# Fused attention and two MLPs: the last tiles of probabilities, phi and v on 128 rows instead of 64

## The reference, cut to what matters

```python
q, k, v: (4, 8, 576, 64)
a = softmax(causal(q @ k.T / 8))                 # per head, 576 x 576
local = a @ v
q_p = where(q > 0, q, exp(q) - 1) + 1            # phi
mem_out = (q_p @ M_prev) / (q_p @ z_prev + 1e-6)
g = sigmoid(beta)                                # per head
attn = g * mem_out + (1 - g) * local
x = attn, heads side by side                     # (2304, 512)
x = (sigmoid(x @ w_gate) * (x @ w_val)) @ w_out  # 512 -> 1536 -> 512
h = x @ w_in                                     # 512 -> 2048
out = (h * clip(h + 3, 0, 6) / 6) @ w_out2       # (2304, 512)
```

## Time and profile before

| | |
|---|---|
| median of 3 runs | 1090.42 us (1088.56 to 1090.96) |
| time of the profiled execution | 1092.04 us |
| its span | 1090.2 us |
| TensorE matmuls, busy | 1066.3 us, 98% |
| TensorE weight loads, busy | 989.9 us, 91% |
| VectorE, ScalarE, GpSimd, busy | 698.4, 629.9, 543.9 us |
| chain that ended last, TensorE's share | 87% |

### The profile page before, as it was taken

The page is one execution under the profiler, slowest core; times in us unless marked ns, Lnnn a source line. Parts: engine busy times, 40 slices in busy tenths (PEclk is TensorE's granted clock), DMA queues, the critical chain, the costliest instruction groups (busy, mean ns, idle before and its releaser), DMA issues.

```text
span 1090.2 us, 20617 instructions
## 1 busy us (share of the span) xinstructions
PE 1066.3 (98%) x6784; PEld 989.9 (91%) x6784; DVE 698.4 (64%) x1521; ACT 629.9 (58%) x1414; POOL 543.9 (50%) x559
## 2 busy tenths in 40 slices
PE   5999999999999999999999999999999999999998
PEld 4668999999999999999999999988888888989887
DVE  5997757768756758767645444466578556664553
ACT  5787676776776767766754443465556343453333
POOL 5887567658766657765644654247881011000000
PEclk9999999999999999999999999999999999999999
DMA  8452442443443343343223335344544544454421
GB/s 187 126 141 65 116 107 65 118 112 82 110 111 94 94 123 95 95 124 96 60 68 97 88 107 175 117 150 140 187 170 148 173 116 119 117 175 121 117 59 58
DMA packets 123596, 125.98 MB, mean 116 GB/s; under 512 B 10352, under 2 KB 89712, under 8 KB 123248
## 3 DMA queue, kind: packets, MB, share of 16 engines
q1 hardware_dynamic: 123216, 121.15, 40.0%
q10 hardware_dynamic: 288, 3.67, 0.9%
HBM read 105.39 MB, written 19.40 MB: 114 GB/s over the span
## 4 chain that ended last, share of the span: by engine, by line
PE 87%; DVE 4%; DMA 2%; issue 2%; ACT 2%; POOL 2%; SPq 1%; DVEq 0%; POOLq 0%; ACTq 0%
PE ps L799 82%; PE ps L840 4%; PE ps L854 1%; DMA stage<-w_val 1%; DMA stage<-w_gate 1%; DVE prob L1536 1%; POOL prob L684 0%; DMA qk_st<-qk_t 0%; DVE q_s L1452 0%; ACT pt_hi L1136 0%; SPq L435 0%; DVE pt_lo L1484 0%; DVE Cb L1728 0%; DVE m_hl L1524 0%; POOL v_hl L651 0%
## 5 line engine op out<-in xcount | busy, mean ns | idle before, releaser
L799 PE MATMUL ps<-x_hi,WG 128*128 128x288 f32 x1536 | 324.2, 297 | 2.2 <-DVE pt_lo L1484 1.1
L799 PEld LDWEIGHTS ps<-x_hi,WG 128*128 128x128 f32 x1536 | 251.3, 188 | 5.2 <-issue 1.9
L799 PE MATMUL ps<-x_lo,WG 128*128 128x288 f32 x768 | 226.2, 295 | 0.0
L799 PE MATMUL ps<-XC,WC 128*128 128x384 f32 x1008 | 202.5, 336 | 2.1 <-DVE Cb L1728 1.7
L799 PEld LDWEIGHTS ps<-XC,WC 128*128 128x128 f32 x1008 | 180.3, 188 | 17.6 <-issue 3.2
L656 POOL TENSOR_TENSOR WG<-stage,WG 128x512 fp32r<-128x512 f32 x96 | 128.2, 1350 | 104.2 <-ACT WG L1164 104.2
L799 PE MATMUL ps<-wo,G_hi 128*128 128x512 f32 x540 | 168.1, 392 | 0.0
L799 PE MATMUL ps<-h_hi,WO 128*128 128x288 f32 x768 | 164.6, 297 | 0.2 <-DVE Y L1703 0.2
L684 POOL TENSOR_SCALAR prob<-prob,rscale 128x128 f32<-128x128 f32 (+4 forms) x160 | 110.9, 711 | 79.4 <-DVE rscale L1496 79.4
L799 PEld LDWEIGHTS ps<-x_lo,WG 128*128 128x128 f32 x768 | 144.3, 188 | 0.5
L1728 DVE TENSOR_TENSOR Cb<-ps,Cb 128x384 f32<-128x384 f32 x168 | 89.0, 554 | 83.3 <-PE ps L799 81.4
(11 more groups left out here) (137 smaller groups left out, 1971.2 us busy)
## 6 DMA issues: line engine op xcount, KB each, us to landing
WC<-w_in_parts SPq DMA_DIRECT2D x112, 256.0 KB, 2.7
stage<-w_out SPq DMA_DIRECT2D x64, 256.0 KB, 2.8
qk_st<-qk_t SPq DMA_DIRECT2D x54, 288.0 KB, 4.4
stage<-w_gate SPq DMA_DIRECT2D x48, 256.0 KB, 3.4
stage<-w_val SPq DMA_DIRECT2D x48, 256.0 KB, 3.3
w_in_parts<-WC SPq DMA_DIRECT2D x42, 256.0 KB, 2.0
qn_st<-q_n SPq DMA_DIRECT2D x16, 256.0 KB, 3.3
w_in_parts<-WC ACTq DMA_DIRECT2D x2, 1792.0 KB, 7.2
```

The costliest lines, as they stand in the source:

```text
L799: return pe.matmul(o, l, r, start=start, stop=stop, skip_group_check=True)
```

## The change

- In `turn_head` the last tile is turned as 128 rows. Each of the five outputs is 128 columns wide, but they still start 64 columns apart, so the second half of one is written over by the first half of the next. The copies out of PSUM read the same columns as before.
- In `turn_phi` the tail is turned as 128 rows. Its tile is now loaded with the last 128 tokens (64 of them for the second time), and what is used is the last 64 columns of the output.
- In `times_v_first` the last tile is multiplied on 128 rows. The rows 64 to 127 of that tile of both `v_first` buffers are cleared once at the start, on GpSimd, and SyncE waits for this (`v_zero`) ahead of the first load of v.
- The clearing of the last tile of `qn_st` is gone.

```diff
-        cleared = [v_st[:, QT - 1, :], qn_st[:, QT - 1, :]]
+        cleared = [v_st[:, QT - 1, :]]
...
             def load_phi(n):
-                load_tiles(qn_st, q_n, n, ld_phi)
+                head = q_n[bass.ds(n, 1), 0:(QT - 1) * P, :].rearrange("a (t p) c -> p (a t) c", p=P)
+                tail = q_n[bass.ds(n, 1), S - P:S, :].rearrange("a p c -> (a p) c")
+                sp.dma_start(qn_st[:, 0:QT - 1, :], head).then_inc(ld_phi, DMA)
+                sp.dma_start(qn_st[:, QT - 1, :], tail).then_inc(ld_phi, DMA)
...
                     for j in two:
                         load_m_first(0, j)
+                    sp.wait_ge(v_zero, 2)
                     load_tiles(v_first[0], v_n, 0, ld_v_first[0])
...
             for ap in cleared:
                 pool.memset(ap.bitcast(F32), 0.0).then_inc(init, 1)
+            for j in two:
+                pool.memset(v_first[j][:, QT - 1, :], 0.0).then_inc(v_zero, 1)
...
                 for k in range(i + 1):
-                    last = pe.transpose(ps[:, turn_bank(r, i), k * rows:(k + 1) * rows],
-                                        prob[odd][0:rows, p_off[i] + k * P:p_off[i] + (k + 1) * P], ident[0:rows, 0:rows])
+                    last = pe.transpose(ps[:, turn_bank(r, i), k * rows:k * rows + P],
+                                        prob[odd][:, p_off[i] + k * P:p_off[i] + (k + 1) * P], ident[:, :])
...
                 for t in (range(QT - 1) if j == 0 else [QT - 1]):
-                    rows = qrows[t]
                     o = t * P if j == 0 else P
-                    last = pe.transpose(ps[:, TURN if j == 0 else turn_bank(r, 0), o:o + rows], phi[0:rows, t, :], ident[0:rows, 0:rows])
+                    last = pe.transpose(ps[:, TURN if j == 0 else turn_bank(r, 0), o:o + P], phi[:, t, :], ident[:, :])
...
                 for k in tiles:
-                    rows = slice(0, qrows[k])
                     for a, b in ((0, P), (P, S)) if k == 0 else ((k * P, S),):
-                        last = mm(head_out(a, b), v_first[n % 2][rows, k, :], pt[rows, k, a:b], False, k == QT - 1)
+                        last = mm(head_out(a, b), v_first[n % 2][:, k, :], pt[:, k, a:b], False, k == QT - 1)
...
-                        (phit_hi[:, (QT - 1) * P:S], ps[:, turn_bank(r, 0), P:P + TAIL])
+                        (phit_hi[:, (QT - 1) * P:S], ps[:, turn_bank(r, 0), 2 * P - TAIL:2 * P])
```

More of the change, by code:

```diff
@@ L232, in attention_and_mlps @@
         ld_qk, ld_v, ld_phi, ld_m, ld_beta = [sem(x) for x in ("ld_qk", "ld_v", "ld_phi", "ld_m", "ld_beta")]
-        init, m_zero = sem("init"), sem("m_zero")
+        init, m_zero, v_zero = sem("init"), sem("m_zero"), sem("v_zero")
         g_e, g_1, g_r, gates = sem("g_e"), sem("g_1"), sem("g_r"), sem("gates")
@@ L1142, in move_phi @@
                 cols = slice(0, (QT - 1) * P) if i == 0 else slice((QT - 1) * P, S)
-                src = ps[:, TURN, 0:(QT - 1) * P] if i == 0 else ps[:, turn_bank(None, 0), P:P + TAIL]
+                src = ps[:, TURN, 0:(QT - 1) * P] if i == 0 else ps[:, turn_bank(None, 0), 2 * P - TAIL:2 * P]
                 act.activation(phit_first[:, cols], src, ACT.Copy).then_inc(moved_act, 1)
@@ L1473, in move_lo @@
                     cols = slice(0, (QT - 1) * P) if i == 0 else slice((QT - 1) * P, S)
-                    src = ps[:, TURN, 0:(QT - 1) * P] if i == 0 else ps[:, turn_bank(r, 0), P:P + TAIL]
+                    src = ps[:, TURN, 0:(QT - 1) * P] if i == 0 else ps[:, turn_bank(r, 0), 2 * P - TAIL:2 * P]
                     dst, hi = phit_lo[:, cols], phit_hi[:, cols]
```

## The result

The changed kernel takes 1085.23 us (median of 6 runs, 1083.96 to 1085.61), the kernel before 1090.29 us in the same comparison. The ratio is 0.9954, with a 95% interval of 0.9941 to 0.9967: 5.0 us faster, between 3.6 and 6.4. The forecast was 7.2 us and 1083.2 us; the gain is 0.7 of that. The time lies inside the wide range of 1079.5 to 1087, and 0.2 us outside of 1081.5 to 1085.0, the range of the forecast's own case.

The account below looks back on a forecast made before the run. TensorE was taken to bound the kernel, with VectorE also busy in the opening. 4.5 us from 97 us on plus 2.7 in the opening, 7.2 in all, off 1090.42 gave 1083.2 us; range 1079.5 to 1087.

Parts of the forecast that it names:

- the forecast's own case: Gaps go, saving 4.5 us from 97 us on and 2.7 in the opening; 1081.5 to 1085.0 us, 53 in 100.
- the two slower rivals: Small groups' gap stays, turns only lengthen: 1097.4 us, 4 in 100; turns wait for overlapping writes: 1103 us, 3 in 100.
- the opening gives nothing: First 97 us: VectorE's order of work sets the pace, TensorE only waits longer; 1085.9 us, 12 in 100.
- from 97 us on: After the opening: 23 heads at 0.09 and 11 phi tails at 0.24, less two waiting steps; 4.5 us.
- a later wait takes it back: Middle stage: ScalarE's waits for weights give each pair its 0.42 us back as waiting; about 1089 us, 8 in 100.
- The opening's term: First 97 us: 3.93 us of TensorE work from heads, phi and v, counted at TensorE's 68.6% chain share; 2.7 us.

Follow-up runs that it names:

- Experiments 1, 7 and 8: 1: only heads' turns on 128 rows, 1090.0 us; 7: VectorE's h_val ahead of a low part, kernel after, 1081.35 us; 8: same, kernel before, 1086.25 us.
- before_again: The kernel before run once more with no edit, for a second trace and as a measure of noise; ratio 0.9998 against itself.
- v alone: Only v's tail in the opening goes to 128 rows, with its clears and SyncE's wait, against the kernel before; 1089.5 us, ratio 0.9997.

## Why the prediction was right, and where it was wrong

The mechanism of the gain was right: small turns are shorter but each visit to 64 rows costs a gap of 0.29 to 0.30 us, and the change takes away one for each head, one for each pair (phi) and one for each tail of v in the opening. The prices were near: 0.07 us a head where 0.09 was forecast, 0.15 in the opening and 0.28 a pair in the middle stage for phi (0.24), 0.29 for v (0.24). Neither of the two slower rivals came true: the gap went, and overlapping writes cost at most the 0.004 us a turn between 0.115 and 0.111. Nor did "the opening gives nothing", though its 1085.9 is nearer to the 1085.23 than the forecast is: its repeating pairs got 0.57 us shorter. That the forecast is off by 2.0 us has other reasons.

Both terms of the sum came out smaller. The term "from 97 us on", 4.5 us, is 4.2 by the repeating distance, 2.2 to 4.6 by pairs of traces, and some 3.2 if the opening's 1.8 us are taken from the 5.0 of the runs. It rested on TensorE being busy for 477.53 of 480 us and on two places with a wait. Two things were wrong in this:
- A wait of 0.12 us on h_val stood in the repeating pairs and in no table of matmuls' waits: their records overlap, so a short idle time hides inside a busy share of 99%. It took the gain of one head of two, 0.08 us a pair, 0.9 us over eleven. Experiments 1, 7 and 8 show it. In a pair of the change it is half made up, for phi's part gained 0.30 us and not 0.24: 0.38 of the 0.42 us that were forecast.
- At the end of a batch ScalarE and VectorE have more to do, and TensorE waited for them there before the change too, by 0.16 and 0.24 us in before_again. Part of a pair's gain turns into waiting: four waits of 0.2 to 0.5 us for the low parts, 1.5 us in the first trace after and 1.6 in the second, against 1.1 and 0.4 before. This is the rival "a later wait takes it back", which was given 8 in 100 for the whole; a part of it came true, some 0.8 us by the waits; against the first trace of before, with 1.8 us of waits in all, nothing of it shows. It was forecast with late weights as the cause. In the case shown ScalarE waited 0.16 us for them and VectorE was held for 2.35 us by another part, so weights aren't the whole of it; which work of a batch's end decides was not tried.

The opening's term, 2.7 us, was too large by 0.9: the pairs that repeat gained 0.57 us each and 1.8 us in all, and no gain of the first pair shows. It counted the gains of five pairs of phi's tail, nine heads and eight tails of v, less 31%. For a pair that repeats the work that left is 0.58 + 0.15 + 0.15 = 0.88 us, and 0.57 of it, 65%, was passed on. That this is near the share of 69% is luck: v's tail was passed on nearly whole (0.5 of 0.58 us a pair), the heads' mostly (0.12 of 0.15), phi's not at all, since TensorE waits for VectorE's maximum just behind it. A share of the chain says how much is TensorE's, not which of its instructions.

Open: v alone gained 1.5 us in the repeating pairs of its trace, and 0.3 us (at most 1.3) in the runs. The three parts by themselves add up to 0.8 + 2.3 + 0.3 = 3.4 us, within their intervals of the 5.0 of the whole. How much of the missing 2.2 us (7.2 forecast, 5.0 measured) belongs to the opening and how much to the middle stage is known only to about 1 us.

## What to carry to other kernels

A lone product on fewer rows in a stream of full ones isn't cheap because it is small: look at the distance between the full ones on both sides, and pad the small one where the padding costs less than the gap. Before a gain on the busiest engine is summed up, look behind each place for the next instruction that waits, also by a tenth of a microsecond. Read the waits of the weight loads beside those of the matmuls, and compare the length of a repeating piece with the sum of its parts. Take a second trace before a sum over a long stage is called a gain: here two of the same kernel differed by 2.1 us in 460. If such a wait is found, reorder the engine that causes it first; here two exchanged instructions of VectorE, and one wait moved on TensorE, brought 3.5 to 3.9 us, more than the forecast of 1.4 to 2.4 and nearly as much as the change.

## What the runs showed of the hardware

Entering and leaving 64 rows costs TensorE 0.29 us around five turns and 0.30 around one, so it is paid for a visit and not for an instruction. A turn of 64 rows and columns stood 0.071 us from the next, one of 128 stood 0.111 to 0.115, also where each wrote over half of the columns that the one ahead had written.
